# Chunk 0's seven tap products: two of them on GpSimd, tap weights in PSUM, no filling matmuls, a new order of transposes

## What is computed

```python
w = exp(weight_gen - max(weight_gen, axis=-1))
w = w / (sum(w, axis=-1) + 1e-9)                 # 7 weights for each token and head
x_pad = concatenate([zeros(6 tokens), x])        # for each of the 2 sequences
att = einsum('bshk,bskhg->bshg', w, windows_of_7(x_pad))      # 24 features in a head
h = maximum(att @ w_in, 0);  y = (h * h) @ w_out              # 192 -> 2048 -> 192
h = y @ w_in2;  out = (h * clip(h + 3, 0, 6) / 6) @ w_out2    # 192 -> 2048 -> 192
```

## Time and profile before

| | before |
|---|---|
| median of 3 runs | 1124.87 us (1124.64 to 1124.95) |
| profiled execution | 1124.62 us, of which the span from first to last instruction is 1122.7 us |
| TensorE matmul busy | 1117.6 us (100%) |
| TensorE weight load busy | 1109.4 us (99%) |
| VectorE busy | 907.1 us (81%) |
| ScalarE busy | 668.9 us (60%) |
| GpSimd busy | 3.1 us |
| first real matmul starts | 12.48 us after the span's start |

### The profile page before, as it was taken

How to read it: one execution, slowest core, us unless ns; L and a number is a source line. 1 busy time by engine, 2 the same in 40 slices (tenths; PEclk the granted TensorE clock), 3 DMA queues, 4 the chain that set the end, 5 groups by cost and what they waited for, 6 DMA issues and landing times.

```text
span 1122.7 us, 25690 instructions
## 1 busy us (share of the span) xinstructions
PE 1117.6 (100%) x10028; PEld 1109.4 (99%) x10028; DVE 907.1 (81%) x986; ACT 668.9 (60%) x746; POOL 3.1 (0%) x10
## 2 busy tenths in 40 slices
PE   9999999999999999999999999999999999999998
PEld 8998999999999999999999999999999999999998
DVE  8788796987979789697887978879788796986565
ACT  7986556565565565646556555565556556565554
POOL 1000000000000000000000000000000000000000
PEclk9999999999999999999999999999999999999999
DMA  7221002020120201103020030200302002010211
GB/s 215 85 66 36 6 16 63 4 74 7 25 53 4 75 6 42 40 0 76 5 65 16 0 77 4 68 13 0 77 4 71 10 14 63 0 39 4 57 16 30
DMA packets 83575, 42.87 MB, mean 38 GB/s; under 512 B 58268, under 2 KB 76700, under 8 KB 83544
## 3 DMA queue, kind: packets, MB, share of 16 engines
q1 hardware_dynamic: 83416, 42.21, 14.5%
q10 hardware_dynamic: 128, 0.22, 0.1%
HBM read 29.42 MB, written 11.40 MB: 36 GB/s over the span
## 4 chain that ended last, share of the span: by engine, by line
PE 99%; SPq 0%; DMA 0%; ACT 0%; issue 0%; DVEq 0%; DVE 0%
PE h_ps L1175 46%; PE y_ps L1186 30%; PE y_ps L1194 20%; PE y_ps L1207 2%; DMA stage<-in_moe_w_in_dram 0%; PE h_ps L1032 0%; SPq L348 0%; PE y_ps L1032 0%; PE y_ps L1425 0%; SPq L356 0%; ACT win L484 0%; ACT xt L513 0%; PE y_ps L1437 0%; PE h_ps L1327 0%; SPq L360 0%
## 5 line engine op out<-in xcount | busy, mean ns | idle before, releaser
L1175 PE MATMUL h_ps<-xt,win 64*128 64x512 f32 x4550 | 1033.6, 386 | 0.0
L1175 PEld LDWEIGHTS h_ps<-xt,win 64*128 64x128 f32 x4550 | 807.6, 184 | 2.3
L1186 PE MATMUL y_ps<-hid_hi,wout 64*128 64x512 f32 x1984 | 529.6, 386 | 0.0
L545 ACT ACTIVATE hid_hi<-hid 128x1024 fp32r<-128x1024 f32 x240 | 255.1, 1063 | 328.7 <-DVE hid L862 161.4
L871 DVE TENSOR_TENSOR hid_lo<-hid,hid_hi 128x1024 fp32r<-128x1024 f32 x253 | 309.5, 1223 | 146.9 <-ACT hid_hi L545 140.7
L1186 PEld LDWEIGHTS y_ps<-hid_hi,wout 64*128 64x128 f32 x1984 | 364.5, 184 | 1.2
L1186 PE MATMUL y_ps<-hid_lo,wout 64*128 64x512 f32 x992 | 304.2, 386 | 0.0
L1194 PE MATMUL y_ps<-hid_hi,wout 64*128 64x512 f32 x992 | 303.9, 386 | 0.0
L1194 PE MATMUL y_ps<-hid_lo,wout 64*128 64x512 f32 x992 | 303.9, 386 | 0.0
L1186 PEld LDWEIGHTS y_ps<-hid_lo,wout 64*128 64x128 f32 x992 | 182.4, 184 | 1.1 <-DVE hid_lo L846 0.3
L1194 PEld LDWEIGHTS y_ps<-hid_hi,wout 64*128 64x128 f32 x992 | 182.5, 184 | 0.7
(11 more groups left out here) (105 smaller groups left out, 407.1 us busy)
## 6 DMA issues: line engine op xcount, KB each, us to landing
xwin<-in_x_dram SPq DMA_DIRECT2D x14, 960.0 KB, 6.1
by_feature<-stage SPq DMA_DIRECT2D x52, 96.0 KB, 2.0
out_dram<-outs SPq DMA_DIRECT2D x240, 16.0 KB, 1.5
out_dram<-outs SPq DMA_DIRECT2D x240, 8.0 KB, 1.4
stage<-by_feature SPq DMA_DIRECT2D x13, 256.0 KB, 3.1
stage<-in_moe_w_out_dram SPq DMA_DIRECT2D x8, 384.0 KB, 3.6
stage<-in_moe_w_in_dram SPq DMA_DIRECT2D x8, 256.0 KB, 3.3
stage<-in_moe_w_in_dram SPq DMA_DIRECT2D x16, 128.0 KB, 3.7
```

The lines of the kernel that those rows point to most:

```text
L545: act.activation(hi, hid[:, slot], ACT.Copy).then_inc(hi_done, 1)
L1175: return pe.matmul(h_ps[:, s % 2, t, :], win[layer][r, wn, cols], src[r, xn, :], start=bool(rows) and n in (0, SHORT) if start is None els ...
L1186: return pe.matmul(ps[:, 0, :], wout[layer][r, tile, w_cols], src, start=bool(rows) and s == 0 and n == 0, stop=not rows and s == STEPS - ...
```

## The change

Products 1 and 2 of chunk 0 are made by GpSimd, which waits for the softmax, for the own and near parts of the window and for the halo zeros, and signals by a new semaphore `pool_product`. VectorE keeps products 0 (last two tokens), 3, 4, 5 and 6 (in two halves). The norm step of chunk 0 becomes two operations: the weights of the four near taps are written to an SBUF corner (`near_probs`, in `acc`), for GpSimd and ScalarE, and all seven to PSUM (`spread_probs`, in `h_ps`), for VectorE. With chunk 1's window buffer `xwin` as two further buffers, each product has a buffer of its own, and VectorE's waits for free buffers go. TensorE turns the products in the order 0, 3, 1, 4, 5; then come the main features of product 2, of the own part and of product 6, by token pairs, and last the rest features of product 2, the own part and product 6. All `fill` calls are dropped. ScalarE splits weight piece 2 behind `split_first_hi` and not ahead of it. The number of prep steps of chunk 0 (`FIRST`) falls accordingly. From chunk 1 on nothing changes.

```diff
+            pool.wait_ge(prep_done, prep_value(0, "norm"))
+            pool.wait_ge(x_own_loaded, 16)
+            pool.wait_ge(x_near_loaded, 32 * B)
+            pool.wait_ge(halo_zeroed, B)
+            for m in POOL_TAPS:                       # (1, 2)
+                tap = TAPS - 1 - m
+                pool.tensor_tensor(products[m]..., xwin_first[:, tap * D:(tap + J) * D]...,
+                                   near_probs[:, :, tap - NEAR:tap - NEAR + 1].broadcast_to([P, JH, GROUP]),
+                                   ALU.mult).then_inc(pool_product, 1)
...
             own_products()
-            for n in range(3):
+            for n in range(2):
                 split_piece(n)
             split_first_hi(xt[1])
-            for n in (3, 4):
+            for n in (2, 3, 4):
                 split_piece(n)
...
             def tap_products():
-                dve.wait_ge(prep_done, prep_value(0, "norm"))
+                dve.wait_ge(prep_done, prep_value(0, "spread"))
                 dve.wait_ge(x_own_loaded, 16)
                 product(0, 1)
                 dve.wait_ge(x_near_loaded, 32 * B)
                 dve.wait_ge(halo_zeroed, B)
-                for m in range(1, TAPS - 1):
-                    if m == 1 + HALO // 2:
-                        dve.wait_ge(x_far_loaded, 32 * B)
-                    if m >= len(products):
-                        dve.wait_ge(product_turned, m - len(products) + 1)
-                    product(m)
-                dve.wait_ge(product_turned, TAPS - len(products))
+                product(3)
+                dve.wait_ge(x_far_loaded, 32 * B)
+                product(4)
+                product(5)
                 product(TAPS - 1, 0)
                 product(TAPS - 1, 1)
...
+                if isinstance(c, int) and c == 0:
+                    near = probs_of[:, :, NEAR:TAPS]
+                    done(dve.tensor_tensor(near_probs, near, wrec..., ALU.mult))
+                    done(dve.tensor_tensor(spread_probs, e, wrec..., ALU.mult))
+                    return
...
-                for m in range(TAPS - 1):
+                for m in (0, 3, 1, 4, 5):
...
-                    if m in (1, 2, 4):
-                        fill()
...
+                pe.wait_ge(pool_product, 2)
+                turn_rows(late, 0, OLD, 0, False, False)
+                pe.wait_ge(own_made, 1)
+                turn_rows(own_part, 0, OLD, 0, False, False)
+                pe.wait_ge(prep_done, prep_value(0, f"mul{TAPS - 1}"))
+                turn_rows(last, 0, OLD, 0, False, True).then_inc(main_turned, 1)
+                turn_rows(late, 0, NEW, 0, False, False)
+                pe.wait_ge(prep_done, prep_value(0, f"mul{TAPS - 1}", 1))
+                turn_rows(last, 0, NEW, 0, False, True).then_inc(main_turned, 1)
+                turn_rows(late, 0, range(J), 1, False, False).then_inc(product_turned, 1)
+                turn_rows(own_part, 0, OLD, 1, False, False)
+                turn_rows(last, 0, OLD, 1, False, True)
+                turn_rows(last, 0, NEW, 1, False, True).then_inc(att_turned, 1)
```

More of the change, by code:

```diff
@@ L71, in conv_mlp_kernel @@
     NPREP = len(PREP)
-    FIRST = len(SOFTMAX) + TAPS + 1
+    POOL_TAPS = (1, 2)
+    FIRST_OPS = SOFTMAX + ["spread"] + [f"mul{m}" for m in range(TAPS) if m not in POOL_TAPS]
+    FIRST = len(FIRST_OPS) + 1
     SLOTS = TAPS + 1
+    NEAR = TAPS - 3
     TURNS = ["turn_main", "turn_rest"]
@@ L170, in conv_mlp_kernel @@
         free_hid = hid[:, :, :, :].rearrange("p a b n -> p (a b n)")
-        products = [acc[:, :], prod[:, 0, :], prod[:, 1, :], free_hid[:, 0:J * D], free_hid[:, J * D:2 * J * D]]
+        products = {0: acc[:, :], 1: xwin[:, 0:J * D], 2: xwin[:, J * D:2 * J * D], 3: prod[:, 0, :], 4: prod[:, 1, :],
+                    5: free_hid[:, 0:J * D], 6: free_hid[:, J * D:2 * J * D]}
+        near_probs = acc[:, 0:JH * (TAPS - NEAR)].rearrange("p (n k) -> p n k", k=TAPS - NEAR)
         own_part = free_hid[:, 2 * J * D:2 * J * D + JHALF * D]
@@ L183, in conv_mlp_kernel @@
         h_ps = ctx.enter_context(nc.psum_tensor("h_ps", [P, 2, PAIR, N], fp32))
+        spread_probs = h_ps[:, 1, 0, 0:JH * TAPS].rearrange("p (n k) -> p n k", k=TAPS)
         y1_ps = ctx.enter_context(nc.psum_tensor("y1_ps", [P, 2, N], fp32))
@@ L204, in conv_mlp_kernel @@
         own_made = sem("own_made")
+        pool_product = sem("pool_product")
         product_turned = sem("product_turned")
@@ L272, in prep_value @@
             if isinstance(c, int) and c == 0:
-                return (SOFTMAX.index(op) if op in SOFTMAX else len(SOFTMAX) + int(op[3:]) + half) + 1
+                return FIRST_OPS.index(op) + half + 1
             if isinstance(c, int) and c == 1:
@@ L476, in _ @@
             pool.memset(xwin_first[PB:PB + 1, 0:HALO * D], 0.0).then_inc(halo_zeroed, 1)
+            pool.wait_ge(prep_done, prep_value(0, "norm"))
[4 more added lines that the diff above has]
+                tap = TAPS - 1 - m
+                pool.tensor_tensor(products[m].rearrange("p (n g) -> p n g", g=GROUP),
+                                   xwin_first[:, tap * D:(tap + J) * D].rearrange("p (n g) -> p n g", g=GROUP),
+                                   near_probs[:, :, tap - NEAR:tap - NEAR + 1].broadcast_to([P, JH, GROUP]),
+                                   ALU.mult).then_inc(pool_product, 1)
         @block.scalar
@@ L506, in own_products @@
                                          xwin_first[:, HALO * D + n * GROUP:HALO * D + (n + 1) * GROUP], ACT.Copy,
-                                         scale=probs_of[:, n, TAPS - 1:TAPS])
+                                         scale=near_probs[:, n, TAPS - 1 - NEAR:TAPS - NEAR])
                 ins.then_inc(own_made, 1)
@@ L761, in product @@
                 done(dve.tensor_tensor(
-                    products[m % len(products)][:, toks.start * D:toks.stop * D].rearrange("p (n g) -> p n g", g=GROUP),
+                    products[m][:, toks.start * D:toks.stop * D].rearrange("p (n g) -> p n g", g=GROUP),
                     xwin_first[:, (tap + toks.start) * D:(tap + toks.stop) * D].rearrange("p (n g) -> p n g", g=GROUP),
-                    probs_of[:, toks.start * HEADS:toks.stop * HEADS, tap:tap + 1].broadcast_to([P, count * HEADS, GROUP]),
+                    spread_probs[:, toks.start * HEADS:toks.stop * HEADS, tap:tap + 1].broadcast_to([P, count * HEADS, GROUP]),
                     ALU.mult))
             def tap_products():
-                dve.wait_ge(prep_done, prep_value(0, "norm"))
+                dve.wait_ge(prep_done, prep_value(0, "spread"))
                 dve.wait_ge(x_own_loaded, 16)
@@ L814, in softmax_norm @@
                 dve.wait_ge(prep_done, prep_value(c, "recip"))
+                if isinstance(c, int) and c == 0:
+                    near = probs_of[:, :, NEAR:TAPS]
+                    done(dve.tensor_tensor(near_probs, near, wrec[:, :].unsqueeze(2).broadcast_to([P, JH, TAPS - NEAR]), ALU.mult))
+                    done(dve.tensor_tensor(spread_probs, e, wrec[:, :].unsqueeze(2).broadcast_to([P, JH, TAPS]), ALU.mult))
+                    return
                 done(dve.tensor_tensor(e, e, wrec[:, :].unsqueeze(2).broadcast_to([P, JH, TAPS]), ALU.mult))
@@ L1128, in multiply @@
                 for n in range(count):
[L1129 to L1133, removed]
+                    pe.matmul(h_ps[:, 1, 1, 0:P], square, square, start=True, stop=True)
             def turn_rows(src, row0, rows, part, start, stop):
@@ L1148, in turn_products @@
                 OLD, NEW = range(JHALF), range(JHALF, J)
-                for m in range(TAPS - 1):
-                    src = products[m % len(products)]
-                    pe.wait_ge(prep_done, prep_value(0, f"mul{m}"))
+                for m in (0, 3, 1, 4, 5):
+                    src = products[m]
+                    if m in POOL_TAPS:
+                        pe.wait_ge(pool_product, 1)
+                    else:
+                        pe.wait_ge(prep_done, prep_value(0, f"mul{m}"))
@@ L1152, in turn_products @@
                     if m:
-                        turn_rows(src, 0, OLD, 0, m == 1, False)
+                        turn_rows(src, 0, OLD, 0, m == 3, False)
                     turn_rows(src, 0, NEW, 0, m == 0, False)
[L1155 to L1160, removed]
@@ L1161, in turn_products @@
-                    if m in (1, 2, 4):
-                        fill()
[L1163 to L1168, removed]
+                    turn_rows(src, 0, range(J) if m else NEW, 1, m == 0, False).then_inc(product_turned, 1)
@@ new lines, in turn_products @@
+                last, late = products[TAPS - 1], products[2]
+                pe.wait_ge(pool_product, 2)
[6 more added lines that the diff above has]
+                pe.wait_ge(prep_done, prep_value(0, f"mul{TAPS - 1}", 1))
```

## The result

| | before | after |
|---|---|---|
| median of 22 runs each | 1124.74 us | 1123.35 us |
| ratio, 95% interval | | 0.9988 [0.9983, 0.9994] |
| profiled execution, its span | 1124.62, 1122.7 us | 1123.4, 1121.5 us |
| first real matmul | 12.48 | 11.07 |
| VectorE turns to piece 0's low part | 11.52 | 10.01 |

The kernel is 1.39 us faster (0.12%), which is less than 0.2%; the forecast was 1.27 (1123.6 us, from a median of before that was 0.13 us higher). The two profiled executions differ by 1.22 us only: the last store landed 2.3 us after its issue where it had taken 1.9, and what lies ahead of it is 1.5 us earlier. The highest of the 22 runs, 1238.25 us at a mean granted clock of 0.851, is left out of the ratio.

The account below looks back on a forecast made before the run. TensorE bounds 99% of the span, so only the work ahead of its first real matmul counts. That matmul moves from 12.48 to 11.1, gaining 1.4; less 0.1 at the ReLU, 1124.87 - 1.3 = 1123.6 us, bounds 1123.2 to 1124.2.

Parts of the forecast that it names:

- VectorE's chain: Chunk 0's start on VectorE: two full products leave (-1.74), near-tap operation adds 0.20; piece 0's low part 1.54 us earlier.
- PSUM access: VectorE's seven-tap write and weight reads in PSUM: taken as no extra cost, with a bound of +0.5 us on the total.
- GpSimd's chain: GpSimd's two products at chunk 0's start: from 5.95, 1.74 us each, no cost for waits, ready at 7.7 and 9.45.
- Transposes and ScalarE: Ahead of the first real matmul: main features turned at 10.3, high parts from 10.35, matmul at 11.1, rest high part 11.15.
- What is late next: ScalarE's pieces 2 to 4 before step 0's ReLU: moved 0.6 us covered by 0.1; ReLU 14.6, 0.1 of gain let go.
- Moving piece 2 alone would gain some tenths: ScalarE's weight piece 2 at the start: moving only its split gains some tenths, since VectorE's chain ends almost simultaneously.
- Rival 1: TensorE before the first real matmuls: without fills its clock falls to 1.2 GHz, costing 1.5 us, result 1125.1; chance 0.27.
- Rival 2: GpSimd's product and VectorE's seven-tap operation exclude each other: VectorE's chain grows 1.5 us, result 1124.8; chance 0.07.
- Rival 3: GpSimd's products at the start: set the start from 1.8 us each, gain gone from 2.5; chance 0.12 of over 2.2.
- Rival 4: Far landing, piece 4's landing or a stall in the first sums eats most of the gain: 1124.4 us; chance 0.05.

Follow-up runs that it names:

- the run with hardly a warm-up: The changed kernel with 1 instead of 14 warm-up matmuls on TensorE; median 1124.53 us.
- the doubled product: The changed kernel with GpSimd making product 2 once more ahead of product 1; median 1126.03 us, shortest two executions 1124.63 and 1124.69 us.
- the two traces without fills: The kernel before with its fills taken out and nothing else changed, traced twice; median 1125.08 us, ratio 1.0007.

## Why the prediction was right

- **VectorE's chain, -1.54.** It was -1.51 (11.52 to 10.01) although the softmax ended 0.06 later than in the profile of before, and the starts foreseen at 5.97, 6.44 and 9.98 came at 6.00, 6.47 and 10.01. The near weights are three taps (4 to 6), 96 elements, not four and 128 as the text above has it; they cost 0.17. PSUM access took none of the bounds that I had kept for it. The run with all products on VectorE shows that this term carries the gain.
- **GpSimd's chain, ready at 7.7 and 9.45.** It was 9.44, by two errors that cancel. I had its waits at nothing, but the last near transfer of the window held it until 6.42, not 5.95; in the old profile VectorE's product 1 came just behind that landing, at 6.24, so that no idle time showed it. And a product takes 1.51, not 1.74: the affine select's row, counted six times, was too long, and a second operand didn't double it. The prediction's other estimate, 1.69, is too long as well. That 9.45 was met is luck.
- **Transposes and ScalarE.** `main_turned`'s first use at 10.36 against 10.35, first real matmul 11.07 against 11.1, rest high part 11.24 against 11.15. The start of the high parts before was 11.72 by ScalarE's timeline, not 11.82, which is the end of piece 2's split; the forecast doesn't use it. That TensorE would be without a gap from 9.22 I had not said; its slack there is gone, so the next gain has to take away transposes too.
- **What is late next.** Piece 4 was split from 13.58, the ReLU came at 14.56 against 14.6, the low part of step 0 at 16.84 against 16.9. Nothing of the 0.1 that I let go was needed.
- **"Moving piece 2 alone would gain some tenths"** was wrong: it gained nothing alone. The second main high part, not the first, releases TensorE, and it waited for the last half product. What the move brings to the whole is protection from a landing that varies.
- **Rival 1, the clock.** It didn't come in any trace, and the rule behind it failed for these transposes. Its price was too low: its terms, 1.4 and 0.2, add up to 1.6 and not 1.5, and slow transposes alone, which it put at 0.2, set the first real matmul back by 1.6 in the run with hardly a warm-up, since TensorE has few waits left to hide them. Whether the changed kernel has lost a reserve is open. Of the 21 executions in the ratio one, 1124.87 us, has a span that is longer too (1123.1); in another, 1124.21, the span is 1121.3, among the shortest. And the kernel before with piece 2 alone moved, which has all its fills, had one of 1125.72 us beside a median of 1124.67.
- **Rival 2, the mutual hold.** The mechanism is real and larger than its price (VectorE's two products took 2.6 us more), but the order of issue and the PSUM weights avoid it: the seven-tap operation started at 5.57, 0.85 ahead of GpSimd, which the landing held. The prediction didn't see the other place for it: piece 0's low part, at 10.01, comes 0.57 behind GpSimd's end, and with the doubled product it waited.
- **Rival 3, a slow GpSimd.** A product of 1.51 us lies under the 1.8 from which it would set the start; but GpSimd began at 6.42, and from there 1.6 would have done it, so this rival was nearer than it looks. Its price was right in kind: a last product 1.5 to 1.9 us later cost the whole gain.
- **Rival 4, less than it says.** Product 4 followed product 3 without idle time, piece 4 and the first sums held nothing up, and the gain came whole.

## What to carry to other kernels

Where two chains end together, cut both, and look for the second one's end before you price a cut of the first. GpSimd can take elementwise work from VectorE at 1.7 times its duration (1.51 against 0.87 us), if VectorE's operations beside it have at most one SBUF input, as here; an operand moved to PSUM bought 2.5 us here. A short stretch of work at the head of a kernel that is TensorE's for the rest of its length is worth exactly what it shortens, and no more.

## What the runs showed of the hardware

- A full-array 128x128 fp32 matmul between 64-row transposes starts about 0.1 us late and then takes 0.42 us until the next transpose starts, where back to back at 2.4 GHz one costs about 0.23 (two instructions, 0.115 each).
- Transposes alone, behind one warm-up matmul at 1.1 us, raised TensorE's clock from 1.2 to 2.4 GHz, at about 12.0 us where they began at 6.73 us.
- The same 14 warm-up matmuls take 4.75 to 6.20 us, as the step from 1.2 to 2.4 GHz comes early or late; in one trace it came only behind them, at about 7.2 us.
- A VectorE operation with two SBUF inputs that meets a reading GpSimd operation waits for it: 1.59 to 1.81 us instead of 0.68, in three traces.
- The last stores land 1.9 to 2.3 us after their issue in eleven traces and 3.0 to 3.2 us in three (medians of two). Between the two traces without fills it is the only difference found behind the start, and the times are 1124.50 and 1126.21 us.
- Weight piece 2, a load of 256 KB issued at 6.1 to 6.3 us, landed 4.0 to 4.9 us later over the 14 traces.
